# One block for both MLPs, leaf merges first, and unread products in TensorE's waits of round 0

## The reference

```
attention (B 4, H 8, S 768, D 48), per batch and head, over t:
    y[t]  = r[t] @ (state + outer(u * k[t], v[t]))
    state = w[t][:, None] * state + outer(k[t], v[t])
x  = y laid out as 3072 tokens x 384
x  = ((x @ w_a) * (x @ w_b)) @ w_out                 # gated MLP, 384 -> 1536 -> 384
h  = x @ w_in2
g  = max(h, 0) + alpha * min(h, 0)
out = g @ w_out2                                     # leaky MLP, 384 -> 2048 -> 384
```

## Time and profile before

| | |
|---|---|
| median of three runs | 1042.29 us (1041.12 to 1042.53) |
| profiled execution | 1042.79 us |
| its span, first to last instruction | 1040.7 us |
| TensorE, products | 1009.0 us (97%) |
| VectorE | 552.1 us (53%) |
| ScalarE | 294.3 us (28%) |
| GpSimd | 47.7 us (5%) |
| HBM read and written | 47 GB/s over the span |

### The profile page before, as it was taken

One profiled execution on the slowest core, in us unless ns is written; L12 is line 12 of the kernel. 1 busy time (PEld: TensorE's weight loads), 2 busy tenths in 40 slices (PEclk: granted clock), 3 DMA queues, 4 the chain that ended last, 5 costly groups with the idle time before them and its releaser, 6 DMA issues. The chain is left out here.

```text
span 1040.7 us, 29059 instructions
## 1 busy us (share of the span) xinstructions
PE 1009.0 (97%) x12458; PEld 983.2 (94%) x12458; DVE 552.1 (53%) x1146; ACT 294.3 (28%) x620; POOL 47.7 (5%) x37
## 2 busy tenths in 40 slices
PE   5789999999999999999999998999999999999998
PEld 4689999999999999999999998999999999999998
DVE  7376574664645646556432434545555545555553
ACT  3424414224133242241322433322222222222211
POOL 4410020000000000000000003200000000000000
PEclk9989999999999999999999999999999999999999
DMA  7354231301311113011020312110101010101000
GB/s 181 99 140 106 66 106 29 90 25 29 89 52 44 48 52 89 3 53 35 26 59 1 105 62 78 46 46 1 46 1 46 2 45 0 45 0 46 1 24 23
DMA packets 42168, 53.01 MB, mean 51 GB/s; under 512 B 5185, under 2 KB 42049, under 8 KB 42049
## 3 DMA queue, kind: packets, MB, share of 16 engines
q1 hardware_dynamic: 40624, 51.04, 17.3%
q10 hardware_dynamic: 1424, 0.23, 0.2%
HBM read 39.46 MB, written 9.44 MB: 47 GB/s over the span
## 5 line engine op out<-in xcount | busy, mean ns | idle before, releaser
L163 PE MATMUL products<-x_parts,weights_hi 128*128 128x384 f32 x576 | 202.1, 351 | 4.2 <-DVE a_sb L873 3.4
L164 PE MATMUL products<-x_parts,weights_hi 128*128 128x384 f32 x576 | 195.4, 339 | 0.0
L165 PE MATMUL products<-x_parts,weights_lo 128*128 128x384 f32 x576 | 195.2, 339 | 0.0
L1145 DVE TENSOR_SCALAR leaky_low<-leaky_h_ps,leaky_al 128x384 f32<-128x384 f32 x128 | 79.0, 617 | 176.4 <-PE leaky_h_ps L165 176.3
L1007 DVE TENSOR_TENSOR g_sb<-a_g,products 128x384 f32<-128x384 f32 x96 | 53.2, 554 | 200.2 <-issue 116.7
L1097 ACT ACTIVATE leaky_g_hi<-leaky_g_sb 128x384 fp32r<-128x384 f32 x128 | 67.3, 526 | 295.9 <-DVE leaky_g_sb L1150 295.9
L493 ACT ACTIVATE g_hi<-g_sb 128x384 fp32r<-128x384 f32 x96 | 50.3, 524 | 245.6 <-DVE g_sb L1007 245.6
L163 PEld LDWEIGHTS products<-x_parts,weights_hi 128*128 128x128 f32 x576 | 109.0, 189 | 8.8 <-issue 5.3
L164 PEld LDWEIGHTS products<-x_parts,weights_hi 128*128 128x128 f32 x576 | 109.1, 189 | 0.0
L165 PEld LDWEIGHTS products<-x_parts,weights_lo 128*128 128x128 f32 x576 | 109.1, 189 | 0.0
L163 PE MATMUL acc<-g_hi,weights_hi 128*128 128x384 f32 x288 | 97.6, 339 | 1.5 <-ACT x_in L493 1.2
(11 more groups left out here) (84 smaller groups left out, 1777.9 us busy)
## 6 DMA issues: line engine op xcount, KB each, us to landing
k_in<-in_k_dram SPq DMA_DIRECT2D x16, 336.0 KB, 4.0
r_in<-in_r_dram SPq DMA_DIRECT2D x16, 336.0 KB, 5.5
stage<-in_w_out_dram SPq DMA_DIRECT2D x14, 384.0 KB, 3.2
w_v<-in_v_dram SPq DMA_DIRECT2D x16, 288.0 KB, 3.3
y_dram<-x_in SPq DMA_DIRECT2D x8, 576.0 KB, 3.4
x_in<-y_dram SPq DMA_DIRECT2D x8, 576.0 KB, 4.5
out_dram<-leaky_out_sb SPq DMA_DIRECT2D x7, 576.0 KB, 3.3
stage<-in_w_dram SPq DMA_DIRECT2D x10, 336.0 KB, 3.8
```

Of the source, the lines that this page charges most:

```text
L163: pe.matmul(out, w_hi, x_hi, start=first, stop=False)
L164: pe.matmul(out, w_hi, x_lo, start=False, stop=False)
L165: return pe.matmul(out, w_lo, x_hi, start=False, stop=last)
L1145: dve.tensor_scalar(low[f % 2][:, :], h, 0.0, al[:, f:f + 1], ALU.min, ALU.mult).then_inc(low_ready, 1)
```

## The change

- The leaky MLP becomes a class whose parts are called from the gated MLP's block. Its four `h_ps` banks are the gated MLP's product banks in the order 2, 3, 0, 1, and its accumulators are the gated ones. `up(0,0,0)` comes before the last gated `down`, `up(0,0,1)` after it. Its tiles lie where the gated weights were, so writers of that room wait for the last gated products.
- The second block's own GpSimd part is gone: VectorE makes the low parts of the last eight pieces, one each in blocks 1 to 8 of the first tile.
- The output copies wait for a count of their own for each 128 tokens (`block_done`).
- In step 11 VectorE does the merges of the leaf; the four steps of keys and queries come in step 12, after block 0's low part.
- In round 0, TensorE gets unread products: 128 x 256 columns with 48 rows, two after the first stream's leaf and one after the second's, five of 128x384 after each of steps 2 to 8; the ten after step 10 stay.
- Alpha is loaded in the last gated tile.

```diff
@@ TensorE, round 0
-                for step in range(BEFORE_TILES):
-                    if step == PHASES:
-                        keep_clock()
+                def keep_clock_early():
+                    pe.matmul(acc[0][:, 0:BANK // 2], k_scratch[0][0:D, 0:P], k_scratch[0][0:D, 0:BANK // 2], start=True, stop=True)
+                leaf(0, 0)
+                keep_clock_early()
+                keep_clock_early()
+                leaf(0, 1)
+                keep_clock_early()
+                for step in range(1, BEFORE_TILES):
                     attend(step)
+                    if 2 <= step <= 8:
+                        keep_clock(CLOCK_PRODUCTS // 2)
+                    elif step == PHASES - 1:
+                        keep_clock(CLOCK_PRODUCTS)
@@ TensorE, behind the last gated block
+                second.up(pe, 0, 0, 0)
                 down(TILES * F1 - 1)
+                second.up(pe, 0, 0, 1)
+                pe.wait_ge(g_ready, F1 * TILES)
+                pe.wait_ge(x2_copied, TILES)
+                second.tensor_part(pe)
@@ VectorE, attend
                     if phase == 0 and n > 0:
-                        if n == 1:
-                            for j in range(2):
-                                first_step_k(n, j)
-                                step_r(n, j, 0)
                         for j in range(2):
                             merge_leaf(n, j)
...
                     elif phase == 1 and n > 0:
+                        if n == 1:
+                            for j in range(2):
+                                first_step_k(n, j)
+                                step_r(n, j, 0)
                         products_of_w(n, 0, 2)
@@ SP, last gated tile
                     if tile == TILES - 1 and f == X_LOAD:
+                        sp.wait_ge(down_done, F1 * tile + 2)
+                        second.load_alpha(sp)
@@ leaky MLP, VectorE
+                    if first and j == 0 and 1 <= f <= LEAKY_PIECES - AHEAD:
+                        if f == 1:
+                            dve.wait_ge(gated_done, gated_count)
+                        shared.split_lo(dve, GATED_PIECES + AHEAD + f - 1)
@@ leaky MLP, GpSimd
-            for n in range(GATED_PIECES + AHEAD, GATED_PIECES + LEAKY_PIECES):
-                shared.split_lo(pool, n)
@@ leaky MLP, ScalarE, outputs of a tile
-                    act.wait_ge(down_done, F2 * (tile + 1))
-                    act.wait_ge(out_stored[j], 16 * b)
-                    for s in range(KT):
-                        copy(out_sb[j][:, s * DM:(s + 1) * DM], acc[s][:, 0:DM]).then_inc(out_copied, 1)
+                act.wait_ge(self.out_stored[j], 16 * b)
+                for s in range(KT):
+                    if s < KT - 1:
+                        act.wait_ge(self.block_done, (KT - 1) * tile + s + 1)
+                    else:
+                        act.wait_ge(self.down_done, F2 * (tile + 1))
+                    copy(self.out_sb[j][:, s * DM:(s + 1) * DM], self.acc[s][:, 0:DM]).then_inc(self.out_copied, 1)
@@ leaky MLP, TensorE, order of the tile
-                    for f in range(F2 + 2):
-                        if f < F2:
-                            up(b, j, f)
+                for f in range(F2 + 2):
+                    if f < F2 and not (first and j == 0 and f < 2):
+                        self.up(pe, b, j, f)
                     if f >= 2:
                         down(b, j, f - 2)
```

More of the change, by code:

```diff
@@ L290, in front @@
             g_hi_ready, g_lo_ready, down_done, x2_copied = sem("g_hi_ready"), sem("g_lo_ready"), sem("down_done"), sem("x2_copied")
+            second = Leaky(nc, ctx, alpha, out, shared, [products[:, BANK * (j ^ 2):BANK * (j ^ 2) + TT] for j in range(4)], acc)
             def queries_of(n, j):
@@ L1022, in _, with __init__ @@
                         shared.split_x_lo(dve, 0, 0)
-def leaky(nc, alpha, out, shared):
-    with ExitStack() as ctx:
+                second.vector_part(dve, down_done, F1 * TILES)
+class Leaky:
+    def __init__(self, nc, ctx, alpha, out, shared, h_ps, acc):
         def sb(name, shape, dt=F32):
@@ L1035, in sem @@
             return ctx.enter_context(nc.semaphore(f"leaky_{name}"))
-        def bank(name):
-            return ctx.enter_context(nc.psum_tensor(f"leaky_{name}", [P, 512], F32))
+        self.alpha, self.out, self.shared, self.h_ps, self.acc = alpha, out, shared, h_ps, acc
+        self.al = sb("al", [P, F2])
+        self.low, self.g_sb = ring("low", 2, [P, TT]), ring("g_sb", 2, [P, TT])
+        self.g_hi, self.g_lo = ring("g_hi", 4, [P, TT], F32R), ring("g_lo", 4, [P, TT], F32R)
+        self.out_sb = ring("out_sb", 2, [P, KT * DM])
         rest = [sb(f"rest_{part}", [P, (LEAKY_PIECES - AHEAD) * PIECE], F32R) for part in ("hi", "lo")]
@@ L1124, in _ @@
[L1124 to L1151, removed]
-                            shared.split_x_lo(dve, 1 - j, tile + 1)
-                    g_low(F2 - 1, F2 * tile + F2 - 1)
-            over_batches(dve, body)
@@ new lines, in scalar_part, with copy, split_x, body @@
+    def scalar_part(self, act, gated_done, gated_count):
+        shared = self.shared
+        def copy(out_, in_):
+            return act.activation(out_, in_, ACT.Copy)
+        def split_x(j, b):
+            act.wait_ge(self.h_done, from0(F2 * (2 * b + j - 1)))
+            act.sem_inc(self.copy_begun, 1)
+            shared.split_x_hi(act, j, 2 * b + j)
+        act.wait_ge(gated_done, gated_count)
+        def body(b, first, last):
+            for j in range(2):
+                tile = 2 * b + j
+                for f in range(F2):
+                    g = F2 * tile + f
+                    act.wait_ge(self.g_ready, g + 1)
+                    act.wait_ge(self.down_done, from0(g - 3))
+                    copy(self.g_hi[f % 4][:, :], self.g_sb[f % 2][:, :]).then_inc(self.g_hi_ready, 1)
+                    if first and j == 0:
+                        if AHEAD + f < LEAKY_PIECES:
+                            shared.split_hi(act, GATED_PIECES + AHEAD + f)
+                    if f == F2 // 2 and not (last and j):
+                        split_x(1 - j, b + j)
+                act.wait_ge(self.out_stored[j], 16 * b)
+                for s in range(KT):
+                    if s < KT - 1:
[3 more added lines that the diff above has]
+                    copy(self.out_sb[j][:, s * DM:(s + 1) * DM], self.acc[s][:, 0:DM]).then_inc(self.out_copied, 1)
+        over_batches(act, body)
@@ new lines, in up @@
+    def up(self, pe, b, j, f):
+        g = F2 * (2 * b + j) + f
+        shared = self.shared
+        if f == 0:
+            pe.wait_ge(shared.x_ready, 2 * b + j + 1)
+        if is_zero(b) and j == 0 and f % 2 == 0:
+            shared.wait_piece(pe, shared.number["w_in2", f // 2])
+        pe.wait_ge(self.g_ready, from0(g - 3))
+        for k in range(KT):
+            w_hi, w_lo = shared.parts("w_in2", f, k * 2 * P + f % 2 * P)
+            x = slice(k * TT, (k + 1) * TT)
+            product = three_products(pe, self.h_ps[f % 4], w_hi, w_lo, shared.x_hi[j][:, x], shared.x_lo[j][:, x], k == 0, k == KT - 1)
+        product.then_inc(self.h_done, 1)
@@ new lines, in tensor_part, with down, body @@
+    def tensor_part(self, pe):
+        shared = self.shared
+        def down(b, j, f):
+            g = F2 * (2 * b + j) + f
+            pe.wait_ge(self.g_lo_ready, g + 1)
+            if f == 0:
+                pe.wait_ge(self.out_copied, KT * (2 * b + j))
+            if is_zero(b) and j == 0 and f % 2 == 0:
+                shared.wait_piece(pe, shared.number["down of w_in2", f // 2])
+            w_hi, w_lo = shared.parts("down of w_in2", f, f % 2 * DM, DM)
+            for s in range(KT):
+                t = slice(s * P, (s + 1) * P)
+                product = three_products(pe, self.acc[s][:, 0:DM], self.g_hi[f % 4][:, t], self.g_lo[f % 4][:, t], w_hi, w_lo,
+                                         f == 0, f == F2 - 1)
+                if f == F2 - 1 and s < KT - 1:
+                    product.then_inc(self.block_done, 1)
+            product.then_inc(self.down_done, 1)
+        def body(b, first, last):
+            for j in range(2):
+                for f in range(F2 + 2):
+                    if f < F2 and not (first and j == 0 and f < 2):
+                        self.up(pe, b, j, f)
+                    if f >= 2:
+                        down(b, j, f - 2)
+        over_batches(pe, body)
@@ L1199, in program @@
         shared = Shared(nc, ctx, y, [([("w_a", w_a), ("w_b", w_b)], w_out), ([("w_in2", w_in2)], w_out2)])
-        front(nc, ctx, r, k, w, v, constants, y, shared)
-        leaky(nc, alpha, out, shared)
+        front(nc, ctx, r, k, w, v, constants, y, alpha, out, shared)
 def lay_channels(x, np):
```

132 lines of the change are left out of this document (65 added, 67 removed).

## The result

The changed kernel takes 1038.34 us (median of 7 runs, 1036.88 to 1041.41) against 1042.29 (1041.12 to 1043.78) before: ratio 0.9967, 95% interval 0.9952 to 0.9982. It is faster by a little: the gain is 4.0 us where 11.3 were forecast. The time lies at the upper end of the range, but not for the reason that the range was drawn for. The likeliest case, a clock that rises near 22 us, did not happen in the traced execution; it rose at 43.9, and what happened is in the main rival 2, most of which the range was meant to leave out.

What follows compares the result with a forecast made beforehand. TensorE was taken as the bound, with gains only where it idles or runs at its lower clock. 1042.8 - 5.6 - 0.8 - 3.55 - 1.3 = 1031.5, less 0.5 to the runs' median: 1031.0; range 1026 to 1038.5 us.

Steps and rivals of the forecast that it cites:

- The likeliest case: Round 0: the clock rises after the second unread group, near 22 us, -1.3 us; forecast 1031.0, chance 0.50.
- rival 2: Round 0: the unread products never raise the clock, +8.4 in place of -1.3 us, 1040.7; chance 0.15.
- Seam and end: Between the two MLPs TensorE's lost time goes, -5.6 us; at the last output copies one remains exposed, -0.8 us.
- Low parts on VectorE: First leaky tile: eight more pieces on VectorE stay hidden behind TensorE; 0 us, bounds 0 and +1.
- Start of tile 0: Leaf merges first end TensorE's 3.36 us wait, -5.05; VectorE's lateness returns 1.5: -3.55 us, bounds -6.3 and -1.2.
- Round 0: Attention's first round: unread products raise TensorE's clock from 1.2 GHz near 22 us; -1.3 us, bounds -4 and +8.4.
- 1: Round 0: the clock is high from the first level and stays, -4 us, 1028.3; chance 0.20.
- 3: Round 0 already at full clock or limited by VectorE: unread products only add, +2.1 in place of -1.3, 1034.4; chance 0.10.
- 4: Tile 0: VectorE's lag is not worked off, 1.5 us in each of ten blocks, 1044.5; chance 0.05.

Runs made afterwards that it cites:

- e6: e1 with the four first steps of keys and queries ahead of the leaf merges again, as before the change: 1035.48 us, ratio 0.9936.
- e12: e1 with the low parts of the last eight pieces on GpSimd again, as in the kernel before: 1032.66 us, ratio 0.9903.
- e1: The changed kernel without the new unread products of round 0 (the ten of before stay): 1032.05 us, ratio 0.9902.
- e5: e1 with twenty kept products in place of ten between round 0 and the leaf of round 1: 1033.40 us, ratio 0.9912.
- e9: e5 with ScalarE's order in the first tile turned: g_hi of the block before the next weight piece's high part; 1030.91 us, ratio 0.9880.
- e2: The kernel before with only the unread products of round 0 added: 1046.94 us, ratio 1.0053.
- e3: The changed kernel with ten instead of five unread products after each of steps 2 to 8: 1037.66 us, ratio 0.9950.
- e8: The changed kernel with ten unread products after step 2 and two after each of steps 3 to 8: 1033.93 us, ratio 0.9921.

## Why the prediction was wrong

- **Seam and end: right.** Predicted -5.6 and -0.8, 6.4 together; e6 gives 6.7. In the traced execution it was 5.7 and 0.9. The wait for `x2_copied` was taken at 0.2 us and is not there at all.
- **Low parts on VectorE: right**, no cost that e12 could tell from the noise.
- **Start of tile 0: right in size.** Predicted -3.55; e1 against e6 gives -3.4. In the traced changed kernel it is 2.6: the start of `up_b(1)` wins 4.6 us, and 2.0 are lost again up to `down(1)`. The new wait on `g_lo` in block 1 came as predicted (1.5 us; 1.1 in e1, 1.8 in the changed kernel), also the part of it that comes from ScalarE's wait for its load. That this load, and not VectorE alone, would swallow a further gain was not seen; e5 and e9 show it.
- **Round 0: the step that failed.** I took it that "the clock rises after the second group, near 22 us", and counted -1.3; the groups cost +6.3 in the median and +7.7 in the traced execution. The rest of that step was sound: TensorE was at 1.2 GHz whatever the clock digits said, a level with its group took 4.6 us (4.5 predicted), and +8.4 was the bound for a clock that never rises. The clock rose only at 43.9, and at 34.0 in e2; seven groups of five lay before the rise in the one, four in the other, and in neither did the second raise it. Groups of ten did, at 20.9 in e3 and 21.7 in e8, but cost more than they gave. So the time in the range is luck: the gain of 1.3 us was a loss, and the sum stayed inside because the range was 12.5 us wide. The chance of 0.15 for rival 2 was too small. The choice had no row behind it: the one rise before, at 45.5, came after a stretch with 1.8 us of the wide products, and no row of before had groups of them between levels. Nor is it sure that the wide products are what raises the clock: the small ones kept TensorE busy for 84% of 14.6 to 43 us before (24.0 of 28.4 us; the prediction says 90%) without a rise, but in e9 it rose at 36.4 with nothing but them ahead of it. What the clock would have given back to a level beside groups of five, 0.4 to 0.7 us by the prediction, no run measured.
- **Rivals.** 1 was not met in its pure form (the first level at full clock) by any run; from the second level on, e3 has the full clock and shows no gain, but with ten unread products a level. 3 is out, since the levels took 1.60 against 2.79 us by the clock. 4 did not come: of tile 0's blocks one alone has a wait on `g_lo`.
- **What stays open.** Of the 7.7 us, 2.1 are the stop before the last four state products (51.12, no releaser). It is there in the three traces in which these products ran at full clock (2.1, 1.4 in e2, 2.8 in e3), and in no other. In the changed kernel, from 48.7 to 51.2 us one load on the instruction queue is the only large packet (queue, packets, MB, share). That TensorE had run out of instructions would fit, but was not tested, and such loads come every few microseconds in each of the traces. What decides where the clock rises stays open too. The view of that stretch in the changed kernel has this row for the instruction queue:

```profile
q8 instruction: 1, 0.02, 2.2%
```

## What to carry to other kernels

Filler work on the engine that sets the pace is only free when it is shorter than the wait it stands in at the clock that holds then, not at the one hoped for. Before buying a faster engine, ask what its neighbours need for the same step: in e5, a weight piece that waited for its load, in front of `g_hi(0)` in ScalarE's order, gave the whole gain back. Put an operation that waits for a transfer behind the one that others wait for (2.5 us from e5 to e9).

## What the runs showed of the hardware

- The share of 1.00 that the profile prints for the stretches before the first rise of the clock is no reading: the levels take 2.79 us there and 1.60 later, at the same 1.00. The time of a known form tells the clock: 96 level products 2.79 or 1.60 us, five 128x384 products 1.97 or 1.15 us.
- A rise does not come at the same place in every execution: at 34.0 and 43.9 us under the same instructions, and in e5 and e9, whose TensorE has the same program up to 50 us, at 45.4 and 36.4. The rise at 36.4 had only the small products of the attention ahead of it; in the nine other traces without such groups in round 0 the clock did not rise before 44.
- Ten 128x384 products between the first two levels were followed by a rise in both traces that had them (at 20.9 and 21.7 us). Of the two traces with groups of five, none had it before 34.
- VectorE's two-input operations beside GpSimd's: 1.47 and 1.94 us against 0.56 and 0.95 alone.
